# Placing the first expert tile with its rows already transposed, and a block of idle-time matmuls behind it

## What is computed

```
q_pool = q.reshape(B, H, S // 2, 2, D).mean(axis=3)         # B=2, H=8, S=1152, D=64
attn = softmax(q_pool @ k.T / sqrt(D));  x = attn @ v       # x: 1152 tokens x 512
logits = x @ w_gate;  e_idx = argmax(logits, axis=1)        # 8 experts
for e in range(8):
    mask = e_idx == e
    h = maximum(x[mask] @ w1[e], 0);  ye = h @ w2[e]        # 512 -> 1024 -> 512
    out[mask] = gate_w[mask] * eom[mask, e] * ye            # eom: sigmoid of the output gate
h = out @ w_in;  y = (h * tanh(softplus(h))) @ w_out        # 512 -> 2048 -> 512
```

## Time and profile before

| | us |
|---|---|
| Median of 3 runs | 681.33 (681.28 to 682.07) |
| The profiled execution | 681.28 |
| Its span, first to last instruction | 679.5 |
| TensorE matmuls busy | 665.0 (98%) |
| TensorE weight loads busy | 594.0 (87%) |
| VectorE, ScalarE, POOL busy | 508.3, 410.0, 81.3 |

### The profile page before, as it was taken

One profiled execution on the slowest core, in us unless ns is written; L12 is line 12 of the kernel. 1 busy time (PEld: TensorE's weight loads), 2 busy tenths in 40 slices (PEclk: granted clock), 3 DMA queues, 4 the chain that ended last, 5 costly groups with the idle time before them and its releaser, 6 DMA issues.

```text
span 679.5 us, 14727 instructions
## 1 busy us (share of the span) xinstructions
PE 665.0 (98%) x5143; PEld 594.0 (87%) x5143; DVE 508.3 (75%) x1188; ACT 410.0 (60%) x841; POOL 81.3 (12%) x116
## 2 busy tenths in 40 slices
PE   7999999999999999989999999999999999999996
PEld 6789898989889989669999899989988988899995
DVE  5777777777777776676665667577999998887873
ACT  5766676766666666555555565666676655445542
POOL 3313140404040300220000000000000000101001
PEclk9999999999999999999999999999999999999998
DMA  8689959797977600469990752041200000001001
GB/s 192 164 245 242 250 140 249 187 259 176 262 176 206 157 1 2 170 245 386 399 378 18 266 189 105 15 155 45 96 0 1 1 0 1 26 21 47 1 1 46
DMA packets 95351, 93.83 MB, mean 138 GB/s; under 512 B 41920, under 2 KB 70976, under 8 KB 94784
## 3 DMA queue, kind: packets, MB, share of 16 engines
q1 hardware_dynamic: 91536, 84.39, 42.4%
q10 hardware_dynamic: 2320, 4.00, 1.8%
q0 software_dynamic: 1440, 4.72, 1.8%
HBM read 59.80 MB, written 16.78 MB: 113 GB/s over the span
## 4 chain that ended last, share of the span: by engine, by line
PE 87%; DVE 6%; ACT 3%; issue 2%; DMA 1%; POOL 0%; ACTq 0%; DVEq 0%
PE score_banks L1066 14%; PE pvT L821 12%; PE turn L840 11%; PE score_banks L1096 11%; PE score_banks L1081 10%; PE score_banks L792 5%; PE score_banks L793 5%; PE score_banks L1118 4%; PE pvT L1118 4%; PE turn L1118 4%; PE score_banks L798 2%; PE turn L756 2%; PE turn L1053 1%; PE turn L1044 1%; DVE w_out_lo L1742 1%
## 5 line engine op out<-in xcount | busy, mean ns | idle before, releaser
L1166 ACT ACTIVATE prob<-score_banks,nmax 128x1152 f32<-128x1152 f32 x72 | 87.9, 1221 | 53.5 <-DVE nmax L1410 53.5
L840 PE MATMUL turn<-ident,prob 128*128 128x128 f32 x648 | 102.4, 279 | 1.0 <-DVE probT L1471 1.0
L1066 PEld LDWEIGHTS score_banks<-xsT,w_slot 128*128 128x128 f32 x832 | 94.6, 192 | 2.5 <-issue 1.5
L1066 PE MATMUL score_banks<-xsT,w_slot 128*128 x832 | 95.1, 275 | 1.1 <-issue 1.1
L840 PEld LDWEIGHTS turn<-ident,prob 128*128 128x128 f32 x648 | 75.1, 141 | 15.4 <-issue 11.0
L821 PE MATMUL pvT<-probT,v_sb 128*64 128x128 f32 (+1 forms) x1404 | 85.9, 269 | 0.0
L821 PEld LDWEIGHTS pvT<-probT,v_sb 128*64 128x64 f32 x1404 | 69.5, 137 | 11.8 <-issue 11.8
L792 PE MATMUL score_banks<-kT,qT 128*128 128x384 f32 x192 | 70.2, 366 | 1.8 <-DVE kT L1424 1.3
L1639 DVE TENSOR_TENSOR w_lo<-w_slot,w_hi 128x512 fp32r<-128x512 f32 x104 | 69.2, 688 | 3.1 <-ACT w_hi L1304 3.0
L1400 DVE TENSOR_REDUCE nmax_part<-score_banks 128x1 f32<-128x768 f32 x72 | 68.2, 948 | 1.3 <-PE score_banks L793 1.1
L1309 ACT ACTIVATE hT_hi<-score_banks 128x128 fp32r<-128x128 f32 x104 | 28.7, 276 | 61.1 <-PE score_banks L1066 56.6
(11 more groups left out here) (251 smaller groups left out, 1362.5 us busy)
## 6 DMA issues: line engine op xcount, KB each, us to landing
w_slot<-moe_w SPq DMA_DIRECT2D x16, 2048.0 KB, 15.0
slots_dram<-zeros SPq DMA_DIRECT2D x8, 1472.0 KB, 11.6
raw_k<-k SPq DMA_DIRECT2D x16, 288.0 KB, 5.9
v_sb<-v SPq DMA_DIRECT2D x16, 288.0 KB, 4.2
w_in_sb<-moe_w_in SPq DMA_DIRECT2D x2, 2048.0 KB, 7.8
w_out_sb<-moe_w_out SPq DMA_DIRECT2D x2, 2048.0 KB, 9.3
raw_q<-q SPq DMA_DIRECT2D x14, 256.0 KB, 3.8
qT<-q_hi SPq DMA_DIRECT2D x28, 128.0 KB, 2.4
```

The lines of the kernel that those rows point to most:

```text
L840: last = pe.transpose(bank[:, j * P:(j + 1) * P], prob[:, s % 2, c * KC + j * P:c * KC + (j + 1) * P], ident[:, :])
L1066: last = pe.matmul(h1_bank[f % 4][:, 0:P], w1_e[:, d, f * P:(f + 1) * P], xsT[:, d, bass.ds((t % XS_RING) * P, P)], start=(d == 0), stop=( ...
L1166: act.activation(prob[:, s % 2, :].rearrange("p (c n) -> p c n", c=NC), scores[s % 2][:, :, 0:KC], ACT.Exp, bias=nmax[:, s:s + 1], accum_o ...
```

## The change

`place_first` swaps its operands. The stationary operand is now a 128 x 128 block of `x_tok`, the moving one is `onehot[:, t, :]`, and the product is the transposed block at once. Each of the nine tiles takes four matmuls of 128 columns instead of one of 512, into four banks (1 to 4 of `score_banks`, 128 columns of each). Tile 0 is split, and only two of its blocks stand ahead of the logits' transposes. The tensor `placed`, its two copies, the four transposes, the two copies behind them and three semaphores are gone; one copy of ScalarE reads the four blocks and writes `xsT`. Behind the last `place_first` stand twelve instructions without a reader: six transposes of the identity, three float32r matmuls of 192 columns and three of 256. On SyncE the wait for `xs_stored` stands ahead of the row number's load. The count that `copy_xs` waits for rises by one, because the first tile now posts `xs_filled` too.

```
-        first_fill = score_banks[:, 1, :]
-        placed_bank = [pvT, turn[0]]
+        first_fill = score_banks[:, 1:1 + DT, 0:P]
...
             sp.wait_ge(x_written, NIT * GB)
+            sp.wait_ge(xs_stored, 16 * TPH)
             sp.wait_ge(rows_ready, 1)
             row = sp.value_load(tile_rows[0:1, 1:2], min_val=0, max_val=(DRAM_TILES - 1) * P)
-            sp.wait_ge(xs_stored, 16 * TPH)
             sp.dma_start(stage[:, :], slots_dram[bass.ds(row, P), :]).then_inc(stage_landed, 16)
...
-            def place_first(t):
+            def place_first(t, parts):
                 pe.wait_ge(onehot_ready, t + 1)
-                return pe.matmul(first_fill, onehot[:, t, :], x_tok[:, t, :], start=(t == 0), stop=(t == TPH - 1))
+                for d in parts:
+                    last = pe.matmul(first_fill[:, d, :], x_tok[:, t, d * P:(d + 1) * P], onehot[:, t, :],
+                                     start=(t == 0), stop=(t == TPH - 1))
+                return last
...
-            place_first(0)
+            place_first(0, (0, 2))
             pe.wait_ge(logits_copied, 2)
...
-            place_first(1)
+            place_first(0, (1, 3))
+            place_first(1, range(DT))
             late_ranks()
             for t in range(2, TPH):
-                last = place_first(t)
-            last.then_inc(first_placed, 1)
-            for half in range(2):
-                pe.wait_ge(placed_copied, half + 1)
-                for m in range(HALF):
-                    last = pe.transpose(placed_bank[half][:, m * P:(m + 1) * P],
-                                        placed[:, (half * HALF + m) * P:(half * HALF + m + 1) * P], ident[:, :])
-                last.then_inc(placed_turned, 1)
+                last = place_first(t, range(DT))
+            last.then_inc(xs_filled, 1)
+            keep_warm(WARM_BEHIND // 2, pvT)
+            for cols in (192, 256):
+                for m in range(3):
+                    pe.matmul(pvT[:, 0:cols], qT[:, 1, 1, 0:P], qT[:, 1, 1, P:P + cols], start=True, stop=True)
...
-            act.wait_ge(first_placed, 1)
-            for half in range(2):
-                cols = slice(half * HALF * P, (half + 1) * HALF * P)
-                act.activation(placed[:, cols], first_fill[:, cols], ACT.Copy).then_inc(placed_copied, 1)
-            for half in range(2):
-                act.wait_ge(placed_turned, half + 1)
-                last = act.activation(xsT[:, half * HALF:(half + 1) * HALF, 0:P],
-                                      placed_bank[half][:, 0:HALF * P].rearrange("p (d n) -> p d n", d=HALF), ACT.Copy)
-            last.then_inc(xs_copied, 1)
+            act.wait_ge(xs_filled, 1)
+            act.activation(xsT[:, :, 0:P], first_fill, ACT.Copy).then_inc(xs_copied, 1)
```

More of the change, by code:

```diff
@@ L166, in build @@
         hT_lo = sb("hT_lo", [P, FT1, P], F32R, hT_at + FT1 * P * 4)
-        placed = sb("placed", [P, D], F32, hT_at)
         y_sb = sb("y_sb", [P, D], F32, hT_at + 2 * FT1 * P * 4)
@@ L300, in build @@
         zeros_ready = sem("zeros_ready")
-        first_placed = sem("first_placed")
-        placed_copied = sem("placed_copied")
-        placed_turned = sem("placed_turned")
         tail_zeroed = sem("tail_zeroed")
@@ L414, in build @@
         warm_bank = score_banks[:, 2, :]
-        WARM_BEFORE, WARM_BETWEEN, WARM_FIRST = 20, 8, 8
+        WARM_BEFORE, WARM_BETWEEN, WARM_FIRST, WARM_BEHIND = 20, 8, 8, 12
         FIRST_Q, FIRST_TAIL = NC, NC + 1
@@ L1270, in _ @@
                 scale(t)
-            act.wait_ge(first_placed, 1)
-            for half in range(2):
-                cols = slice(half * HALF * P, (half + 1) * HALF * P)
-                act.activation(placed[:, cols], first_fill[:, cols], ACT.Copy).then_inc(placed_copied, 1)
-            for half in range(2):
-                act.wait_ge(placed_turned, half + 1)
-                last = act.activation(xsT[:, half * HALF:(half + 1) * HALF, 0:P],
-                                      placed_bank[half][:, 0:HALF * P].rearrange("p (d n) -> p d n", d=HALF), ACT.Copy)
-            last.then_inc(xs_copied, 1)
+            act.wait_ge(xs_filled, 1)
+            act.activation(xsT[:, :, 0:P], first_fill, ACT.Copy).then_inc(xs_copied, 1)
             def copy_xs(t, bank, at):
-                act.wait_ge(xs_filled, t)
+                act.wait_ge(xs_filled, t + 1)
                 act.activation(xsT[:, :, bass.ds(at * P, P)], bank[:, :].rearrange("p (d n) -> p d n", d=DT), ACT.Copy
```

## The result

The changed kernel took 685.05 us (median of 7 runs, 683.42 to 685.79) beside 681.28 us before (680.63 to 682.47): ratio 1.0053, 95% interval 1.0036 to 1.0069. It is 3.8 us slower. The kernel before has two groups of times in every set of runs: up to 681.8 us with a mean granted clock of 0.997 to 0.999, and 681.9 to 683.2 us with 0.995 or 0.996. The changed kernel's profiled execution took 686.05 us, its span is 684.3, 4.8 longer than before.

The account below looks back on a forecast made before the run. TensorE, busy 98% of the span, bounds the kernel, with its first expert matmul held by register steps behind the transposes. Placements, copy and fillers allow an earlier start: 681.33 - 1.15 = 680.2 us, range 679.7 to 681.8.

Parts of the forecast that it names:

- part 2: Late placements on TensorE: five tiles as 40 passes take 4.70 us instead of 4.56, ending at 293.24 instead of 293.45.
- marks: End of VectorE's chain behind the logits' transpose, releasing TensorE's late placements: forecast at 288.54 instead of 288.89.
- Rival (c): TensorE's clock falls in the first expert tile because fillers don't count as work: 682.8 us, chance 0.05.
- Part 1: Logits' transpose on TensorE starts at about 284.45, 0.35 us earlier, and VectorE's chain behind it moves by that.
- Part 3: One ScalarE copy of 0.60 us and register steps done ahead: first expert matmul could start at about 294.2.
- Part 4: Twelve fillers ahead of the first expert matmul: transposes 0.65 us, float32r matmuls 0.68; array free at 294.41.
- rival (a): The 192-column float32r fillers run at plain float32's rate: gain 0.70, 680.6 us, chance 0.30.
- The cap: Expert stage: block 5 waits for VectorE's bank, so a first matmul before 294.60 gives nothing; gain at most 1.18.
- rival (d): VectorE's chain and copies give over 1.4 us, since transposes and bank waits overlap better: 679.8 us, chance 0.09.
- SyncE: Row number's load follows the nine writes: DMA goes out at 298.7, 2.1 us to spare, costing nothing.

Follow-up runs that it names:

- e1: The changed kernel without its twelve fillers (the instructions without a reader), on chip 9: 679.43 us, ratio 0.9972.
- i2: The kernel before with each 512-column placement issued as four matmuls of 128 columns, operands as before, on chip 3: 687.45 us, ratio 1.0088.
- e4: The changed kernel with 84 instead of 20 idle transposes at the very start, on chip 9: 685.36 us, of which 5.8 are longer start.
- i1: The changed kernel without its twelve fillers, run again on chip 3: 686.5 us, ratio 1.0067.
- f3: The changed kernel with the six transposes as its only fillers, the six float32r matmuls left out, on chip 12: 683.85 us.
- e3: The changed kernel with POOL's five late indirect DMAs held until the first expert tile's rows are copied, on chip 9: 685.32 us, ratio 1.0069.
- h3: The changed kernel with one long-satisfied wait in POOL's code ahead of its first late scatter, on chip 13: 684.16 us, ratio 1.003.

## Why the prediction was wrong

**The step that failed is part 2**, "As 40 passes they take 0.105 + 39 x 0.111 + 0.27 = 4.70". The spacing was taken from the earlier trace rows, a stream of 64 in the expert stage, with no scatter of POOL beside it. On chip 9 the step holds: in e1 50 passes of the passage end at 286.81 + 6.11 = 292.92, and the 40 late ones start 0.11 apart. In the changed kernel's trace they took from 288.77 to 298.47, 9.70 us. I had asked what narrower passes cost the array, and took it as given that four times the records would reach it as fast as they could run; no rival asked that either. i2 shows that the narrow passes alone bring the standstill; what holds them up stays open.

**The sum of it**, by the prediction's own points: first expert matmul forecast at 294.41; marks 0.23 later than forecast (288.77 for 288.54), placements 9.70 - 4.70 = 5.00 more, fillers 300.69 - 298.27 = 2.42 instead of 1.33, so 1.09 more: 300.73, measured 300.69.

**Rival (c)** had the clock fall, and it fell, but not because of the fillers. With the fillers at full pace (e4) the clock stays at full, and in i1, which has none, it falls behind the standstill as well. Ahead of the fall TensorE had been busy for 1.87 of 5.0 us in the changed kernel and 1.90 in i1; in f3's trace, with 2.17, it did not fall. At 0.61 over 4.4 us it was at 1.2 GHz for 4.4 x 0.39 / 0.5 = 3.4 us, which loses 1.7; f3, where it didn't fall, has a span 2.8 us shorter, fewer fillers included. e3, which has no standstill, shows a fall as well, behind its wait of 3.6 us for a DMA (0.84 from 300.7 to 310). So the fall follows TensorE's idle time, not the fillers. Chance 0.05 for it, and 0.08 for slower in all, left the result outside.

**Part 1 holds for the transpose, not for the marks.** The transpose started at 284.10, forecast 284.45. Of the 0.72 against before, some 0.3 lies ahead of this passage already and is not explained. The marks were to come by as much earlier; in e1 they did (first late weight load at 288.18), but in the changed kernel `slot` was 0.45 late, the first late placement came at 288.77, and all but 0.12 of the 0.72 was gone.

**Part 3 holds.** One copy over four banks took 0.60. The sequencer's lead, 16 passes by the earlier trace rows, was 17 in e1; its check stood at 293.6 and the first expert matmul at 293.86, where the forecast without fillers was 294.2 with marks 0.36 later.

**Part 4 holds**, rival (a) doesn't: in e4 the twelve fillers took 299.94 - 298.58 = 1.36, forecast 1.33; the six float32r ones 0.79, forecast 0.68.

**The cap was too tight.** A start before 294.60 was to give nothing. In e1 it started 1.92 us earlier than before, and at the last expert tile 1.79 of it was left (the transposes of y_sb at 463.85 and 465.64). VectorE's block 1 (e1, timeline) came 0.77 earlier, not 0.35:

```profile
298.26 0.28 DVE L1630 SCALAR_TENSOR_TENSOR hT_lo<-score_banks,hT_hi 128x128 fp32r<-128x128 f32 x1
```

It is the earlier trace rows's 299.03. So where nothing stands still the change is worth more than the 1.15 forecast: 1.4 with its fillers (e4, less its longer start) and 1.5 without them (e1). That is the size of rival (d), and its reason too, that bank waits overlap better than forecast.

**SyncE holds in what it costs.** No wait for `stage` or weights appears in the changed kernel. The DMA went out at 298.15 (297.86 in e1), not at 298.7. e3 shows that the time to spare is small: with the last five scatters held until the copy, the same read cost 3.6 us.

## What to carry to other kernels

Splitting matmuls into narrow passes can cost the array almost nothing (the late placements took 4.7 us in e1 and 4.56 before) and still multiply the records that must reach it (here by four); where other engines and many small DMAs are busy, look first at whether "issue" gaps open between matmuls that wait for nothing, and at how far the sequencer is ahead. Put the kernel in question itself beside every group of variants on the same chip, since the absence of a disturbance in a variant may belong to the chip or the job. Work given to an idle TensorE so as to keep its clock up is no help against a standstill ahead of it.

## What the hardware showed that was not expected

- TensorE can stand still inside a stream of matmuls with all operands ready: single passes or pairs 0.72 or 1.43 us apart, over 3.5 to 5 us. In the changed kernel the granted clock is 1.00 up to its end, and in the 4.4 us behind it TensorE runs at 1.2 GHz for 3.4.
- It ends within 0.1 us of the start of the last transfers of POOL's last scatter (changed kernel, i1, i2, f2).
- One program took 679.43 us (679.13 to 680.05) in one job, on chip 9, and 686.5 (683.75 to 687.39) in another, on chip 3, while the kernel before differed by 0.7 us between the same jobs.
- ScalarE's copy in h3 started 3.1 us after the matmul that it waited for had ended, and VectorE's `slot` came 0.4 us late, 4 us ahead of the standstill. Both wait for a signal of TensorE.
- Three float32r matmuls of 192 columns and three of 256 took 0.79 us together at full clock, 0.13 apart (e4).
